# Products of ones ahead of an attention loop: 23 narrow ones replaced by four wider ones

## The reference, cut to what matters

```
def _attn_ref(r, k, v, w, u):                    # S = 768 positions
    for t in range(S):
        cur = einsum('bhd,bhe->bhde', u * k_t, v_t)
        y[:, :, t] = einsum('bhd,bhde->bhe', r_t, state + cur)
        state = w * state + einsum('bhd,bhe->bhde', k_t, v_t)

def _moe_ref(x, phi, w1, w2):                    # d, c: softmax of x @ phi over rows and columns
    slot_out[e] = relu((d.T @ x)[e] @ w1[e]) @ w2[e]
    return c @ slot_out

def _moe2_ref(x, w_gate, w1, w2):                # one expert for each token
    out[mask] = gate_w[mask] * (relu(x[mask] @ w1[e]) @ w2[e])
```

## Time and profile before

| | us |
|---|---|
| runs shown (three) | 281.08, 278.13, 280.01; median 280.01 |
| profiled execution, its own time | 278.49 |
| its span, first to last instruction | 276.7 |
| mean granted TensorE clock, share of full | 0.978 |

### The profile page before, as it was taken

One profiled execution on the slowest core, in us unless ns is written; L12 is line 12 of the kernel. 1 busy time (PEld: TensorE's weight loads), 2 busy tenths in 40 slices (PEclk: granted clock), 3 DMA queues, 4 the chain that ended last, 5 costly groups with the idle time before them and its releaser, 6 DMA issues.

```text
span 276.7 us, 10448 instructions
## 1 busy us (share of the span) xinstructions
PE 259.0 (94%) x4505; PEld 218.1 (79%) x4505; DVE 154.6 (56%) x322; ACT 89.0 (32%) x175; POOL 30.6 (11%) x45
## 2 busy tenths in 40 slices
PE   7969799999999998999999889999999999999992
PEld 6747687888787884433479589999999999999991
DVE  7957688889898874435031486532522524425213
ACT  1234355545545443030230363222222222222200
POOL 3321122222212215000000000000000000000000
PEclk9999999999999999999995799999999999999998
DMA  6964899999999999999408300030020300300303
GB/s 162 364 232 146 268 347 359 404 389 404 403 391 366 322 415 418 428 402 422 201 0 308 149 2 0 0 115 0 29 85 0 114 0 0 114 0 7 109 0 120
DMA packets 16260, 55.30 MB, mean 200 GB/s; under 512 B 1872, under 2 KB 5136, under 8 KB 15344
## 3 DMA queue, kind: packets, MB, share of 16 engines
q1 hardware_dynamic: 13152, 43.90, 42.3%
q10 hardware_dynamic: 3088, 11.14, 10.6%
HBM read 50.31 MB, written 4.72 MB: 199 GB/s over the span
## 4 chain that ended last, share of the span: by engine, by line
PE 89%; DVE 4%; issue 3%; ACT 1%; POOL 0%; DVEq 0%; POOLq 0%
PE ps L1199 12%; PE ps L1198 12%; PE ps L1200 12%; PE ps L931 8%; PE ps L954 6%; PE ps L969 6%; PE ps L978 5%; PE ps L943 5%; PE ps L1183 4%; PE ps L1069 4%; PE ps L1091 4%; PE ps L983 3%; PE ps L893 3%; PE ps L1038 2%; PE ps L1140 1%
## 5 line engine op out<-in xcount | busy, mean ns | idle before, releaser
L828 DVE SCALAR_TENSOR_TENSOR hl<-ps,hh 128x512 fp32r<-128x512 f32 x48 | 32.9, 690 | 57.2 <-ACT hh L570 57.2
L1199 PE MATMUL ps<-w2l,hh 128*128 128x384 f32 x192 | 64.6, 336 | 0.0
L1198 PE MATMUL ps<-w2h,hh 128*128 128x384 f32 x192 | 64.4, 335 | 0.0
L1200 PE MATMUL ps<-w2h,hl 128*128 128x384 f32 x192 | 64.2, 335 | 0.0
L570 ACT ACTIVATE hh<-ps 128x512 fp32r<-128x512 f32 x48 | 28.6, 598 | 74.2 <-PE ps L1183 74.2
L1199 PEld LDWEIGHTS ps<-w2l,hh 128*128 128x128 f32 x192 | 36.0, 188 | 1.6
L1198 PEld LDWEIGHTS ps<-w2h,hh 128*128 128x128 f32 x192 | 36.0, 188 | 0.7
L1200 PEld LDWEIGHTS ps<-w2h,hl 128*128 128x128 f32 x192 | 36.1, 188 | 0.0
L437 POOL TENSOR_TENSOR kt<-intk,kttab 128x384 f32<-128x384 f32 x24 | 24.2, 1007 | 71.3 <-DVE rkb L642 61.0
L642 DVE TENSOR_TENSOR rkb<-ind,tab 128x1024 f32<-128x1024 f32 x24 | 29.7, 1240 | 0.3 <-DMA ind<-dmaj 0.2
L931 PE MATMUL ps<-rkb 64*64 64x128 f32 x768 | 27.3, 273 | 0.0
(11 more groups left out here) (165 smaller groups left out, 302.5 us busy)
## 6 DMA issues: line engine op xcount, KB each, us to landing
ind<-dmaj SPq DMA_DIRECT2D x22, 512.0 KB, 7.5
wearly<-wa ACTq DMA_DIRECT2D x21, 512.0 KB, 7.0
intk<-tmaj SPq DMA_DIRECT2D x24, 384.0 KB, 6.5
wearly<-wa SPq DMA_DIRECT2D x4, 1536.0 KB, 10.2
out<-acc SPq DMA_DIRECT2D x5, 768.0 KB, 3.6
wlate<-wa SPq DMA_DIRECT2D x4, 768.0 KB, 9.3
wlate<-wa SPq DMA_DIRECT2D x2, 1536.0 KB, 11.5
wmid<-wa SPq DMA_DIRECT2D x1, 1536.0 KB, 9.0
```

The lines of the kernel that those rows point to most:

```text
L828: v.scalar_tensor_tensor(out=hl[:, f % 4, :], in0=ps[:, f % 4, :], scalar=0.0, in1=hh[:, f % 4, :].bitcast(F32), op0=ALU.max, op1=ALU.subt ...
L1198: mm(o, a_h, w2h[:, f, :], start=(f == 0), stop=False)
L1199: mm(o, a_h, w2l[:, f, :], start=False, stop=False)
L1200: ins = mm(o, a_l, w2h[:, f, :], start=False, stop=(f == KF - 1))
```

## The change

The helper `warm` loses its width. A new helper, `wide`, makes one product of ones with 512 columns, the 128 columns of `ones` read four times over, into a whole PSUM bank. Seven products of 128 columns become two of 512, in two banks; sixteen of 32 columns become one of 512 and one of 128. The products are left as float32.

```
-            def warm(n, bank, width=P):
+            def warm(n, bank):
 
                 for _ in range(n):
-                    mm(ps[0:width, bank, 0:width], ones[:, 0:width], ones[:, 0:width], start=True, stop=True)
+                    mm(ps[:, bank, 0:P], ones[:, :], ones[:, :], start=True, stop=True)
+
+            def wide(bank):
+
+                mm(ps[:, bank, :], ones[:, :], ones[:, :].unsqueeze(1).to_broadcast([P, 4, P]), start=True, stop=True)
 
             pe.wait_ge(consts, 1)
-            warm(7, SC)
+            wide(SC)
+            wide(SC + 1)
             pe.wait_ge(consts, NCONST)
...
             clear(SB + 1, LB)
-            warm(16, SC, NS)
+            wide(SC)
+            warm(1, SC)
             pe.wait_ge(small_in, 4 * 16)
```

## The result

The changed kernel took 279.28 us in the median of 20 runs (276.03 to 280.86), the kernel before 277.90 in the median of 20 (274.81 to 282.0). The ratio is 1.0077, with a 95% interval of 1.0047 to 1.0108: slower by 0.5 to 1.1%, some 2.1 us. The forecast was 0.4% faster. The time itself lies inside the stated range; the sign is the other one.

The account below looks back on a forecast made before the run. TensorE bounds the kernel, with instruction fetches setting the first pass's pace. Three stops in place of four start step 4 at 29.3 rather than 30.35 us, gaining 1.05; median 278.8 us, 0.4% faster, range 276.8 to 281.4.

Parts of the forecast that it names:

- the stated range: Whole kernel: time expected between 276.8 and 281.4 us, to hold 8 in 10 with scatter and rivals.
- the 38 of the count: Loop's first pass: 76 fewer instructions ahead of the loop move each fetch boundary 38 pairs of weight load and product deeper.
- the fifth: End of the first pass: fifth fetch boundary moves about three instructions behind the loop's branch, leaving three stops of four.
- Rivals 1 and 3: Rival 1: fifth boundary is still waited for at the loop's jump, time 280.0, chance 0.15; rival 3 has its own line.
- Rival 2: First pass: stops don't move with the count, or something else late hides them; 280.0 us, chance 0.09.
- mostly hidden: First pass: the skill calls the fetch-crossing cost mostly hidden; prediction said this fails, three of four crossings idling over a microsecond.
- the covers: Ahead of the loop: waits for wk (6.80) and kt (9.71) hide slower wide products; loop still starts at 9.96.
- Two more at 4.55 give 20.85 and 25.4: First pass: second and third stops end at 20.85 and 25.4 us, each fetch taking the mean 4.55 us.
- rival 3: Loop exit: block behind the loop is dropped and fetched again, 2.7 us slower, 282.7, more if DMA queues are full; chance 0.07.
- Forecast of step 4: First pass: step 4 starts at 29.3 us against 30.35 before, a gain of 1.05 us.
- First stop: First pass, line 931 of step 1: the first fetch takes 4.95 us and the stop ends at 16.3 us.
- my 278.8: Whole kernel: forecast median after the change, between 279.0 from the median and 278.4 from the average; chance 0.62.

Follow-up runs that it names:

- e3: Changed kernel, with the loads of intk 4 and ind 5 also waiting for the increments of step 2; median 278.18 us, by ratio 0.2% below before.
- e1_wide_same_count: Kernel before, with wide products in the first group and 21 of 32 columns in the second, again 120 records; time can't be told from before.
- e9_first_group_only: Kernel before, with only the first group changed to two 512-column products, 100 records; slower than before by as much as the whole change.
- e8_changed_again: The changed kernel run once more, nothing altered; late packet, long stop and low clock at the same places within 0.1 us; no total time given.
- e12: Kernel before (120 records), with the loads of intk 4 and ind 5 held until the increments of step 2; step 4 at 31.13 us, no total given.
- e4_second_group_only: Kernel before, with only the second group changed to one 512-column and one 128-column product, 64 records; slower by as much as the whole change.
- e2_narrow_low_count: Kernel before, with four 128-column products in the first group and none in the second, 44 records; 1.75% above before.
- e11_mixed_188: Kernel before, with the first group as one 512-column and 23 16-column products, 188 records ahead of the loop; ratio 1.0136.
- e5: Changed kernel, with the loads of intk 4 and ind 5 no longer waiting for step 1's scores, so issued earlier; ratio 0.9991.
- e10: Kernel before, with the first group as 24 products of 32 columns in place of seven of 128, 188 records; ratio 1.0036.
- e6: Kernel before, with the loads of intk 4 and ind 5 issued earlier, near 13.8 us; step 4 began 0.27 us later, no total given.
- e7: The products of e1_wide_same_count plus 68 semaphore marks behind the two wide products, 188 instructions ahead of the loop; time 2.6% up.

## Why the prediction was wrong

**Right: what the stops are and where they go.** The stops are fetches of instructions in blocks of constant length. By the weight loads they moved by 36 or 37 pairs, close to the 38 of the count (155 to 192, 279 to 315, and in e3 403 to 439), the fifth left the pass, no fetch was waited for at the jump, and none was missing behind the loop (line 989 begins 0.72 us behind its releaser as before, at 107.74). Rivals 1 and 3 didn't come. Rival 2 is refuted: the stops moved, and the 20 records between e1_wide_same_count and e9_first_group_only are worth 1.2 us of the first pass. With it the "mostly hidden" of the Trainium skill (Runtime: NRT & Kernel Launch, section Instruction fetch mechanics) doesn't hold in this stretch.

**Right, narrowly: the covers.** The wide records came 0.85 us apart, the products behind them ended at 6.79 against 6.80 for wk, and the transposes came 0.15 us later. The loop's start moved from 9.96 to 10.12 in this execution and stayed at 9.93 by the weight loads in e8_changed_again, so that is no cost of the change.

**Wrong: "Two more at 4.55 give 20.85 and 25.4".** This is the step that failed. I took the three intervals between stops of the kernel before, 4.21 to 4.77 us, as the duration of a fetch wherever it stands. The one that mattered took 6.96 us (16.65 to 23.61). I had read a late packet as "DMA queues full" for rival 3 only, and had not laid the issue of ind and intk, which hangs on the steps and not on the count, beside the new time of the request. The packet in question was within half a microsecond of their data in the kernel before already. 1.6 us of the excess are these loads, by e3; about 0.8 stay unexplained.

**Missed: the clock.** No part of the sum had a price for a long stop beyond its own length. From the end of the second stop to step 4 the changed kernel takes 9.71 us and e3, with the same instructions and the clock whole, 7.99: the difference of 1.7 us is the half clock, and that although the half-speed stretch hides the third fetch (no stop at pair 440, 0.55 us in e3).

**The sum, as it came out.** Forecast of step 4: 29.3. First stop 0.35 later; second fetch 2.4 longer; what follows it 9.7 in place of 8.45. That makes 33.3. In e3, with the loads away, step 4 came at 29.65, within my 28.6 to 29.8 for both ends of the later fetches: a gain of 0.67 us on the kernel before, where I had 1.05, and of 1.5 on e12, which met a collision of its own. So a gain of the size I had computed is likely but not cleanly measured. The longer fetch and the clock cost more than three times as much: 3.7 us.

**The number.** That 279.28 lies near my 278.8 is luck. I had started from three runs with a median of 280.01; beside the changed kernel the kernel before took 277.90. The error in the starting point and the error in the sign nearly cancelled.

**From step 4 to the end** the loss is 3.1 us at the loop's exit (104.64 against 107.74) and 2.1 us in the comparison of the runs. In the two profiles shown it shrinks among the gates: the first product of the experts' loop comes at 157.71 before and 159.17 after, where the clock was at 0.50 for 10.2 us before and 6.8 after. In e8_changed_again that stretch had 10.2 us as well, and the same product came at 161.64. How long the clock stays low there differs from one execution to the next, and the time goes with the granted clock: the five executions of the changed kernel with a mean clock of 0.989 or 0.990 took 276.03 to 276.97 us, the other fifteen (0.966 to 0.979) 278.12 to 280.86. Whether the change has a part in it, these runs don't settle.

In the experiments the delay at the loop's exit and the difference in time agree within 1 us (e4_second_group_only 2.2 and 2.1, e9_first_group_only 1.9 and 2.0, e3_loads_later -0.7 and -0.5), with two exceptions: e2_narrow_low_count and e11_mixed_188 leave the loop 2.7 and 0.9 us later than the kernel before and are by their ratios 4.9 and 3.8 us slower. No cause was found for that rest.

**Still open:** what sets the rest of the lag between the end of a stop and the next packet. It is 1.6 to 2.0 us in the kernel before, 3.0 in e3 with idle DMA engines, and 1.3 in the changed kernel at half clock (23.61 to 24.94). The half clock alone doesn't make it short: in e4_second_group_only the same lag, at half clock too, is 2.1 (22.48 to 24.55). No run here took it apart.

## What to carry to other kernels

The written-out loop body of this kernel paid for its instructions once, in the first pass (20.4 us against 14.8 for each later one), and there a change of the number of instructions ahead of it, in a place where TensorE had time to spare, moved the fetches against the data loads. Before removing or adding instructions in such a kernel, lay the packets of the instruction queue beside the windows of DMA share: the one that mattered here started 0.4 us ahead of a burst of loads, and ten pairs fewer put it behind. If it must move, try moving the loads with it (an extra wait on the loads of step 1 took the whole loss away here), and put a price on the half clock that a longer stop can bring (1.7 us here).

## What the runs showed of the hardware that was not expected

- In the first pass an instruction packet of 16 KB took 0.9 to 1.4 us and TensorE resumed 1.2 to 1.6 us after its end; from one stop's end to the next it took 4.2 to 4.8 us in the kernel before, 5.3 us in e3 with idle DMA engines, and 7.0 us in the changed kernel with 0.9 MB of loads ahead of the packet.
- Passes two to six took 14.8 us each, before and after, with no instruction packet between 26.4 and 106.7 us in the kernel before: the loop's blocks were fetched once and not again.
- The granted clock fell to the 1.2 GHz level during or right behind each stop of over 3 us (changed kernel twice, e2, e4, e9). For shorter stops the length doesn't tell: it fell with those of 2.27 us (e5), 1.91 and 1.28 (e10) and 1.61 and 1.35 (e11), and not with those of 2.24 (e12), 1.94 (e1, e6) or 1.73 (e3).
- A mark on a semaphore between products is far from free: the 68 of e7 run from 1.3 to 11.6 us, 0.15 us from one to the next, though each record is 51 ns long, and TensorE idled for 6.7 us.
- The products of ones ahead of the loop do serve the clock: e2, with fewer of them, ran its products ahead of the loop and the first ones of step 0 at half speed, although the profile's windows show a clock of 1.00 there, as they do for the first products of every kernel here. At the start of a program durations tell the clock and the column doesn't.
